# Linear attention and two expert layers on one core: the first four attention chunks with full-row instead of half-row matmuls from level 1 on

## Chip, cores and metric

One core of a Trainium2 chip (trn2). The metric is the time of one execution in microseconds of the device, from the first to the last instruction of the program with its start and end around it.

## What is computed

The program computes three layers on 4 x 768 tokens with model width 384, in fp32:

```python
# q, k, v, alpha: [4, 8, 768, 48]; state: [4, 8, 48, 48], zero at the start of each sequence
for t in range(S):
    state = alpha[:, :, t, :, None] * state + np.einsum('bhd,bhe->bhde', k[:, :, t], v[:, :, t])
    y[:, :, t] = np.einsum('bhd,bhde->bhe', q[:, :, t], state)
x = y, heads beside each other                    # [3072, 384]
h = x @ w_in; g = where(h > 0, h, exp(min(h, 0)) - 1); x = g @ w_out     # 384 -> 2048 -> 384
out = sum over e of p[:, e] * (maximum(x @ w1[e], 0) @ w2[e])            # 4 experts, 384 -> 1024 -> 384
```

## The kernel before, in words

**Units and chunks.** The 3072 tokens are 24 chunks of 128; two chunks are a unit. Channels lie on the partitions: a pair of heads takes 128 of them, each head 48 in a half of 64, the rest zero. Weights of the pairs (query t, key s inside a chunk) are found in seven levels: at level l, with h = 2^l, each block of 2h tokens gives the products of its right half's queries and its left half's keys, then the queries of the right halves and the keys of the left halves are multiplied by decays, so that the next level can use them. Decays of level l+1 are products of two of level l (`totals`, L1003, GpSimd).

**The first four chunks** (EARLY, units 0 and 1) come before anything else and have functions of their own; these are what the change touches. TensorE does `early_pairs` (L414), level by level, in each level chunks 0 to 3. For each of the four head pairs there are two matmuls, one per head, on the partitions 0 to 63 and 64 to 127 (a half of the rows each), 128 keys against the 64 right-half queries, into two PSUM banks (`ps_even`, `ps_odd`). Each fp32 matmul is two records in the trace, so a chunk is 16 records. VectorE does `early_queries` (L620, one multiply per unit and level, after both chunks of the unit) and, for levels 0 to 3, `early_masked` (L632): two predicated copies a chunk from PSUM into the weights. GpSimd does `early_keys` (L1029, one multiply per unit and level) and `totals`. ScalarE does levels 4 to 6 of the weights as `early_rectangles` (L827), 8, 4 and 2 small copies a chunk. A level of a chunk waits for queries, keys and the emptied bank of the level before.

**Behind the levels**, TensorE goes on in fixed order (L537 to L551): transposes of the keys (L449), the first state (L438), outer products (L461) and `attend` (L464, L479 and L481) for four chunks; ScalarE copies transposed keys (L856) and outputs into `x_tile` (L865, L867, L881). After attend 3 the expert layers start with the first 512 tokens: per weight block j (48 blocks a tile, six tiles) `hidden` and `output`, three fp32r matmuls (L500 to L502) of 512 columns per product. Weights are loaded by SP (L331), split into high and low parts by ScalarE (L874) and VectorE (L676). The other ten units of attention are spread over the blocks by the table PARTS_AT (L116); they already use full-row matmuls: queries are kept in slots (`QL`, [P, pair, 2, token]), the slot of head 0 with zeros below partition 63 and that of head 1 with zeros above, filled by `expand` (L806, L815), and one matmul of 128 columns serves a pair of heads (`pairs`, L399, L411).

**The queues.** SP issues every transfer in program order: alpha, keys, queries of unit 0 (512 KB each), masks, the same for unit 1, small constants, values, four weight blocks, the blocks of unit 2 (`load_blocks`), then `load_unit(2)`, whose waits for the key transposes and for attend 1 hold weights 4 to 7. The unit-1 queries lie in the buffer `p_rows`, the weights of chunk 2 in the other half of it, those of chunk 3 in `products`.

## Time and profile before

| | |
|---|---|
| median of 3 runs (lowest, highest) | 1410.71 us (1410.6, 1410.97) |
| the profiled execution's own time | 1410.88 us |
| its span, first to last instruction | 1409.1 us |
| TensorE matmul busy | 1386.8 us, 98% |
| TensorE weight load busy (beside it) | 1172.3 us, 83% |
| VectorE, ScalarE, GpSimd busy | 866.3 (61%), 664.7 (47%), 549.9 (39%) us |
| mean granted TensorE clock | 0.999 |
| 0 to 81 us: TensorE, VectorE, ScalarE, GpSimd busy | 70.15, 38.11, 26.66, 45.07 us |
| first matmul, first expert matmul | 7.48, 80.99 us |

The span is cut by the first and last instruction; the execution's time is 1.8 us longer. A row of the trace gives start or count, busy time and, in brackets, the idle time before it and who ended it. Matmul ends are modelled, so a busy TensorE is not one at its peak; for its speed look at how far apart the starts of like records lie, which in the chain of waits is the length given for a group.

### The profile page before, as it was taken

Reading aid. Unit: us, or ns where it says so; the run is one execution under the profiler, and the core shown is the slowest. Engines: PE = TensorE matmul, PEld = TensorE weight load, DVE = VectorE, ACT = ScalarE, POOL = GpSimd, SP = SyncE. Lnnn points to the kernel's source line nnn. Section 1 sums busy time; section 2 is a strip of 40 time slices with the busy share of each in tenths; the row PEclk is TensorE's granted clock in tenths of the full one; section 3 lists DMA queues with packets and bytes.
Section 4 is the critical chain, followed back from the end, with each engine's and each line's share of the span. In section 5 each row is a group of like instructions: output and inputs, shape, how many; then the busy total and the mean of one; then the engine's idle time right before and its main releaser. Section 6 shows DMA issues by size and latency. Waiting matters only on the chain.

```text
span 1409.1 us, 19709 instructions
## 1 busy us (share of the span) xinstructions
PE 1386.8 (98%) x6984; PEld 1172.3 (83%) x6984; DVE 866.3 (61%) x1199; ACT 664.7 (47%) x1187; POOL 549.9 (39%) x517
## 2 busy tenths in 40 slices
PE   7989999999999999999999999999999999999998
PEld 7978888888888888888888888888887888887886
DVE  5278777676556766556756646667655654654443
ACT  0556554436534446643444753443663443563331
POOL 6474383750443761155473153375134421100012
PEclk9999999999999999999999999999999999999999
DMA  5044434235435235424423523523542332343330
GB/s 224 16 160 152 124 103 157 68 88 181 146 91 187 84 90 166 158 79 145 136 79 96 196 91 112 180 80 95 172 152 85 91 97 79 118 126 92 99 101 23
DMA packets 84005, 166.21 MB, mean 118 GB/s; under 512 B 30146, under 2 KB 31683, under 8 KB 83908
## 3 DMA queue, kind: packets, MB, share of 16 engines
q1 hardware_dynamic: 83908, 164.96, 37.8%
q8 instruction: 56, 0.92, 0.3%
q14 instruction: 41, 0.34, 0.1%
HBM read 158.85 MB, written 6.08 MB: 117 GB/s over the span
## 4 chain that ended last, share of the span: by engine, by line
PE 89%; issue 5%; DVE 3%; ACT 2%; POOL 1%; DMA 1%; SPq 0%; POOLq 0%; ACTq 0%; DVEq 0%
PE ps_h L500 13%; PE ps_h L502 12%; PE ps_h L501 12%; PE ps_o L500 12%; PE ps_o L502 12%; PE ps_o L501 12%; PE ps_att L411 4%; PE ps_att L481 3%; PE ps_att L431 2%; PE ps_att L479 1%; PE ps_att L461 1%; PE ps_o L431 1%; DVE w_lo L676 1%; PE ps_att L449 1%; POOL acc L1056 1%
## 5 line engine op out<-in xcount | busy, mean ns | idle before, releaser
L500 PE MATMUL ps_o<-g_hi,w_lo 128*128 128x512 f32 x864 | 348.2, 403 | 1.2 <-DVE g_lo L692 1.2
L676 DVE TENSOR_TENSOR w_lo<-w_stage,w_hi 128x768 fp32r<-128x768 f32 x288 | 322.4, 1120 | 37.8 <-ACT w_hi L874 33.7
L500 PE MATMUL ps_h<-x_hi,w_lo 128*128 128x512 f32 x864 | 337.7, 391 | 7.3 <-DVE g_lo L696 3.7
L502 PE MATMUL ps_o<-g_hi,w_hi 128*128 128x512 f32 x864 | 337.5, 391 | 0.0
L501 PE MATMUL ps_o<-g_lo,w_hi 128*128 128x512 f32 x864 | 336.6, 390 | 0.0
L502 PE MATMUL ps_h<-x_hi,w_hi 128*128 128x512 f32 x864 | 336.4, 389 | 0.0
L501 PE MATMUL ps_h<-x_lo,w_hi 128*128 128x512 f32 x864 | 336.2, 389 | 0.0
L901 ACT ACTIVATE g_hi<-ps_h 128x512 fp32r<-128x512 f32 x192 | 114.8, 598 | 461.9 <-PE ps_h L502 461.2
L696 DVE SCALAR_TENSOR_TENSOR g_lo<-ps_h,g_hi 128x512 fp32r<-128x512 f32 x192 | 132.2, 689 | 235.7 <-ACT g_hi L901 235.4
L268 POOL TENSOR_TENSOR products<-q_block,k_block 128x384 f32<-128x384 f32 x150 | 190.9, 1286 | 136.9 <-DVE scores L613 134.2
L874 ACT CAST w_hi<-w_stage 128x768 fp32r<-128x768 f32 x288 | 239.0, 832 | 1.7
L500 PEld LDWEIGHTS ps_h<-x_hi,w_lo 128*128 128x128 f32 x864 | 162.1, 188 | 45.8 <-issue 6.2
L1056 POOL TENSOR_TENSOR acc<-acc,part 128x512 f32<-128x512 f32 x54 | 72.7, 1375 | 309.6 <-DVE part L722 309.6
L502 PEld LDWEIGHTS ps_o<-g_hi,w_hi 128*128 128x128 f32 x864 | 162.1, 188 | 35.7
L502 PEld LDWEIGHTS ps_h<-x_hi,w_hi 128*128 128x128 f32 x864 | 162.2, 188 | 34.1
L501 PEld LDWEIGHTS ps_h<-x_lo,w_hi 128*128 128x128 f32 x864 | 162.2, 188 | 33.4
L500 PEld LDWEIGHTS ps_o<-g_hi,w_lo 128*128 128x128 f32 x864 | 162.6, 188 | 31.6 <-DVE g_lo L692 2.0
L501 PEld LDWEIGHTS ps_o<-g_lo,w_hi 128*128 128x128 f32 x864 | 162.7, 188 | 30.0
L1027 POOL TENSOR_TENSOR k_level<-k_level,decay 128x256 f32<-128x256 f32 x60 | 39.1, 652 | 287.3 <-PE ps_att L411 287.3
L688 DVE SCALAR_TENSOR_TENSOR elu_out<-elu_exp,ps_h 128x512 f32<-128x512 f32 x96 | 65.8, 686 | 72.0 <-ACT elu_exp L890 72.0
L692 DVE TENSOR_TENSOR g_lo<-elu_out,g_hi 128x512 fp32r<-128x512 f32 x96 | 72.1, 752 | 61.1 <-ACT g_hi L896 61.1
L896 ACT CAST g_hi<-elu_out 128x512 fp32r<-128x512 f32 x96 | 59.6, 620 | 92.1 <-DVE elu_out L688 73.2
(101 smaller groups left out, 1404.4 us busy)
## 6 DMA issues: line engine op xcount, KB each, us to landing
w_stage<-in_w SPq DMA_DIRECT2D x288, 384.0 KB, 3.1
v_tok<-in_v SPq DMA_DIRECT2D x12, 576.0 KB, 5.0
alpha<-in_a SPq DMA_DIRECT2D x12, 512.0 KB, 4.1
k_level<-in_k SPq DMA_DIRECT2D x12, 512.0 KB, 6.1
p_rows<-p_norm SPq DMA_DIRECT2D x6, 1024.0 KB, 8.9
q_low<-in_q SPq DMA_DIRECT2D x11, 512.0 KB, 6.8
out<-acc SPq DMA_DIRECT2D x18, 256.0 KB, 4.3
q_block<-in_q_blocks SPq DMA_DIRECT2D x10, 384.0 KB, 3.7
```

The lines of the kernel that those rows point to most:

```text
L268: return engine.tensor_tensor(dst, q[:, :, 1, i:i + 1, :].broadcast_to([P, pairs, h, D]), k[:, :, 0], ALU.mult)
L500: nc.tensor.matmul(dst, lhs[1], rhs[0], start=first, stop=False)
L501: nc.tensor.matmul(dst, lhs[0], rhs[1], start=False, stop=False)
L502: return nc.tensor.matmul(dst, lhs[0], rhs[0], start=False, stop=last)
L676: nc.vector.tensor_tensor(wl[n % WRING][:], stage[n % STAGE][:], wh[n % WRING][:].bitcast(F32), ALU.subtract).then_inc(w_low, 1)
L688: nc.vector.scalar_tensor_tensor(gt[n % 2][:], ex[n % 2][:], -1.0, ps_h[n % 2][:], ALU.add, ALU.max).then_inc(h_read, 1)
L692: nc.vector.tensor_tensor(gl[n % GS][:], gt[n % 2][:], gh[n % GS][:].bitcast(F32), ALU.subtract).then_inc(g_ready, 1)
L696: nc.vector.scalar_tensor_tensor(gl[n % GS][:], ps_h[n % 2][:], 0.0, gh[n % GS][:].bitcast(F32), ALU.max, ALU.subtract).then_inc(g_ready, 1)
L874: nc.scalar.copy(wh[n % WRING][:], stage[n % STAGE][:]).then_inc(w_hi, 1)
L896: nc.scalar.copy(gh[n % GS][:], gt[n % 2][:]).then_inc(g_hi, 1)
L901: nc.scalar.activation(gh[n % GS][:], ps_h[n % 2][:], ACT.Relu).then_inc(g_hi, 1)
L1056: nc.gpsimd.tensor_tensor(acc[:, m, :], acc[:, m, :], part[k % 2][:], ALU.add).then_inc(acc_added, 1)
```

## The change

For the first four chunks, level 0 stays as it is. Levels 1 to 6 use the slot form: ScalarE copies the dense queries of a unit into zeroed slots after each query update (`early_slots`, the whole of both halves at level 0, only the changed right halves later), and TensorE does one full-row matmul of 128 columns for each pair, 8 records a chunk, into one bank. The predicated copies take 512 columns in one instruction from level 1 on, and level 4 is a masked copy on VectorE instead of small copies on ScalarE; levels 5 and 6 are 2 and 1 copies of ScalarE a chunk. VectorE clears `p_rows` as well, which becomes unit 1's slots; its dense queries move to `acc`, the first key and value to `part`, chunk 2's weights to the block buffers. Keys and queries are loaded by chunk (256 KB each, rows of 512 bytes) in the order chunk 0, alpha 0, chunk 1, masks, alpha 1, chunks 2 and 3. `load_unit(2)` stands ahead of `load_blocks(2)`, which waits for attend 2 (the third), since its buffer holds the weights of chunk 2; weights 4 to 7 are behind both. The diff, without renamed semaphores, index changes and the host's masks:

```diff
+MASKED = 5
...
-        blocks = [sb(f"{name}_block", [P, SUB * D]) for name in "qka"]
+        blocks = sb("blocks", [P, 3, SUB * D])
...
-        mk = sb("masks", [P, LOW, HALF])
-        k0 = acc[0:1, 0, :].rearrange("p (a t) -> p a t", a=PAIRS)
-        v0 = acc[0:1, 1, 0:PAIRS * 2 * D].rearrange("p (a e) -> p a e", a=PAIRS)
-        flat = pb[:].rearrange("p e t -> p (e t)")
-        QE = [QT[:], flat[:, 0:PAIRS * UNIT].rearrange("p (a t) -> p a t", a=PAIRS)]
-        PE_W = [PW[0][:], PW[1][:], flat[:, PAIRS * UNIT:2 * PAIRS * UNIT].rearrange("p (a t) -> p a t", a=HEADS),
-                prods[:].rearrange("p r x -> p (r x)")[:, 0:HEADS * P].rearrange("p (a t) -> p a t", a=HEADS)]
+        mk = sb("masks", [P, MASKED, HALF])
+        k0 = part[0][0:1, :].rearrange("p (a t) -> p a t", a=PAIRS)
+        v0 = part[1][0:1, 0:PAIRS * 2 * D].rearrange("p (a e) -> p a e", a=PAIRS)
+        QE = [QT[:], acc[:].rearrange("p a t -> p (a t)")[:, 0:PAIRS * UNIT].rearrange("p (a t) -> p a t", a=PAIRS)]
+        QS = [QL[:], pb[:].rearrange("p e (s t) -> p e s t", s=2)]
+        PE_W = [PW[0][:], PW[1][:]]
+        PE_W += [b[:].rearrange("p r x -> p (r x)")[:, 0:HEADS * P].rearrange("p (a t) -> p a t", a=HEADS) for b in (blocks, prods)]
...
+        q_in, e_in = sem("q_loaded"), [sem(f"early_q_k_loaded_{g}") for g in range(EARLY)]
@@ -261,7 +262,7 @@
@@ -282,31 +283,36 @@
             def load_blocks(u):
                 if u > LEAD:
                     sp.wait_ge(prod, NPROD * (u - LEAD))
+                else:
+                    sp.wait_ge(y_done, 3)
                 for i, d in enumerate((qb_d, kb_d, ab_d)):
-                    sp.dma_start(blocks[i][:], d[u]).then_inc(block_in[i], 16)
+                    sp.dma_start(blocks[:, i, :], d[u]).then_inc(block_in[i], 16)
 
             def load_unit(u):
                 s = u % 2
                 if u >= 2 * LEAD:
                     sp.wait_ge(k_low, LOW * (u - 2 - LEAD) + 1)
                     sp.wait_ge(q_low, LOW * (u - 2 - LEAD) + 1)
-                elif u >= LEAD:
+                else:
                     sp.wait_ge(e_k, early_unit(u - LEAD, 0))
                     sp.wait_ge(e_q, early_unit(u - LEAD, 0))
-                if u >= LEAD:
-                    sp.wait_ge(td_ready, LEVELS * (u - 2) + 1)
+                sp.wait_ge(td_ready, LEVELS * (u - 2) + 1)
                 sp.dma_start(TD[0][s][:], a_d[u]).then_inc(a_in[s], 16)
-                if u >= LEAD:
-                    sp.wait_ge(kt_done, 2 * (u - 1))
+                sp.wait_ge(kt_done, 2 * (u - 1))
                 sp.dma_start(KL[s][:], k_d[u]).then_inc(k_in[s], 16)
-                if u < LEAD:
-                    sp.dma_start(QE[u], q_d[u]).then_inc(e_q_in[u], 16)
-                    return
                 if u == LEAD:
                     sp.wait_ge(y_done, 2)
                 else:
                     sp.wait_ge(q_slots, u - LEAD)
                 sp.dma_start(QT[:], q_d[u]).then_inc(q_in, 16)
+
+            def load_early(g):
+                u, t = g // 2, slice(P * (g % 2), P * (g % 2 + 1))
+                sp.dma_start(KL[u][:, :, t], k_d[u][:, :, t]).then_inc(e_in[g], 16)
+                sp.dma_start(QE[u][:, :, t], q_d[u][:, :, t]).then_inc(e_in[g], 16)
+
+            def load_alpha(u):
+                sp.dma_start(TD[0][u][:], a_d[u]).then_inc(a_in[u], 16)
 
             def load_v(u):
                 if u >= 2:
...
 
-            load_unit(0)
+            load_early(0)
+            load_alpha(0)
+            load_early(1)
             sp.dma_start(mk[:], masks_d).then_inc(masks_in, 16)
-            load_unit(1)
+            load_alpha(1)
+            load_early(2)
+            load_early(3)
             sp.dma_start(k0, k0_d).then_inc(first_in, 16)
             sp.dma_start(v0, v0_d).then_inc(first_in, 16)
             sp.dma_start(eye[:], eye_d).then_inc(eye_in, 16)
@@ -354,8 +364,8 @@
             for n in range(STAGE):
                 load_w(n)
             sp.dma_start(pr_raw[:], probs_d).then_inc(p_raw_in, 16)
+            load_unit(LEAD)
             load_blocks(LEAD)
-            load_unit(LEAD)
             for n in range(STAGE, 2 * STAGE):
                 load_w(n)
             sp.wait_ge(p_step, 4)
@@ -413,27 +423,30 @@
 
             def early_pairs(g, l):
                 u, c = divmod(g, 2)
+                t = slice(P * c, P * (c + 1))
                 if l == 0:
-                    pe.wait_ge(k_in[u], 16)
-                    pe.wait_ge(e_q_in[u], 16)
-                else:
-                    pe.wait_ge(e_q, early_unit(u, l - 1))
+                    pe.wait_ge(e_in[g], 32)
+                else:
+                    pe.wait_ge(e_slot, early_unit(u, l - 1))
                     pe.wait_ge(e_k, early_unit(u, l - 1))
-                    if l <= LOW:
+                    if l <= MASKED:
                         pe.wait_ge(e_mask, early_chunk(g, l - 1))
                     else:
-                        pe.wait_ge(e_rect, early_chunk(g, l - 1 - LOW))
-                t = slice(P * c, P * (c + 1))
+                        pe.wait_ge(e_rect, early_chunk(g, l - 1 - MASKED))
                 for pr in range(PAIRS):
-                    for sd, ps_g in enumerate((ps_even[g], ps_odd[g])):
-                        r = slice(HALF * sd, HALF * (sd + 1))
-                        right = QE[u][r, pr, t].rearrange("p (m two h) -> p m two h", two=2, h=1 << l)[:, :, 1, :]
-                        last = nc.tensor.matmul(ps_g[:, HALF * pr:HALF * (pr + 1)], KL[u][r, pr, t], right, start=True, stop=True)
+                    if l == 0:
+                        for sd, ps_g in enumerate((ps_even[g], ps_odd[g])):
+                            r = slice(HALF * sd, HALF * (sd + 1))
+                            right = QE[u][r, pr, t].rearrange("p (m two) -> p m two", two=2)[:, :, 1]
+                            last = nc.tensor.matmul(ps_g[:, HALF * pr:HALF * (pr + 1)], KL[u][r, pr, t], right, start=True, stop=True)
+                    else:
+                        right = QS[u][:, pr, :, t].rearrange("p s (m two h) -> p s m two h", two=2, h=1 << l)[:, :, :, 1, :]
+                        last = nc.tensor.matmul(ps_even[g][:, pr * P:(pr + 1) * P], KL[u][:, pr, t], right, start=True, stop=True)
                 last.then_inc(e_step, 1)
 
             def first_state():
                 pe.wait_ge(first_in, 32)
-                pe.wait_ge(e_rect, early_chunk(0, LEVELS - 1 - LOW))
@@ -634,11 +647,16 @@
                 dve.wait_ge(e_step, early_chunk(g, l))
                 if l:
                     dve.wait_ge(e_mask, early_chunk(g, l - 1))
-                for sd, ps_g in enumerate((ps_even[g], ps_odd[g])):
-                    dst = weights(g).rearrange("p (a s) (m two h) -> p s a m two h", s=2, two=2, h=h)[:, sd, :, :, 1, :]
-                    mask = mk[:, l, :].rearrange("p (m h) -> p m h", h=h).unsqueeze(1).broadcast_to([P, PAIRS, HALF // h, h]).bitcast(U32)
-                    src = ps_g[:, 0:PAIRS * HALF].rearrange("p (a m h) -> p a m h", a=PAIRS, h=h)
-                    last = nc.vector.copy_predicated(dst, mask, src)
+                mask = mk[:, l, :].rearrange("p (m h) -> p m h", h=h).unsqueeze(1)
+                if l == 0:
+                    for sd, ps_g in enumerate((ps_even[g], ps_odd[g])):
+                        dst = weights(g).rearrange("p (a s) (m two) -> p s a m two", s=2, two=2)[:, sd, :, :, 1]
+                        last = nc.vector.copy_predicated(dst, mk[:, 0, :].unsqueeze(1).broadcast_to([P, PAIRS, HALF]).bitcast(U32),
+                                                         ps_g[:, 0:PAIRS * HALF].rearrange("p (a m) -> p a m", a=PAIRS))
+                else:
+                    dst = weights(g).rearrange("p a (m two h) -> p a m two h", two=2, h=h)[:, :, :, 1, :]
+                    last = nc.vector.copy_predicated(dst, mask.broadcast_to([P, HEADS, HALF // h, h]).bitcast(U32),
+                                                     ps_even[g][:].rearrange("p (a m h) -> p a m h", a=HEADS, h=h))
                 last.then_inc(e_mask, 1)
...
 
-            for buffer in (QL, SC[0], SC[1]):
+            for buffer in (QL, pb, SC[0], SC[1]):
                 nc.vector.memset(buffer[:], 0.0).then_inc(q_clear, 1)
...
                 for u in range(LEAD):
                     early_queries(u, l)
-                    if l < LOW:
+                    if l < MASKED:
                         for c in range(2):
                             early_masked(2 * u + c, l)
-            dve.wait_ge(q_clear, 3)
+            dve.wait_ge(q_clear, 4)
@@ -824,16 +842,29 @@
                     last = nc.scalar.copy(QD[g % 2][r, :, 0:HALF], QL[r, :, sd, P * (g % 2):P * (g % 2) + HALF])
                 last.then_inc(q_left, 1)
 
+            def early_slots(u, l):
+
+                act.wait_ge(e_q, early_unit(u, l))
+                if l:
+                    act.wait_ge(e_slot, early_unit(u, l - 1))
+                else:
+                    act.wait_ge(q_clear, u + 1)
+                for sd in range(2):
+                    r = slice(HALF * sd, HALF * (sd + 1))
+                    new, old = QS[u][r, :, sd, :], QE[u][r]
+                    if l:
+                        new, old = [x.rearrange("p a (m two h) -> p a m two h", two=2, h=1 << l)[:, :, :, 1, :] for x in (new, old)]
+                    last = nc.scalar.copy(new, old)
+                last.then_inc(e_slot, 1)
+
             def early_rectangles(g, l):
                 h = 1 << l
                 act.wait_ge(e_step, early_chunk(g, l))
                 act.wait_ge(cleared, CLEARS)
-                for sd, ps_g in enumerate((ps_even[g], ps_odd[g])):
-                    src = ps_g[:, 0:PAIRS * HALF].rearrange("p (a t) -> p a t", t=HALF)
-                    dst = weights(g).rearrange("p (a s) t -> p s a t", s=2)[:, sd]
-                    for m in range(HALF // h):
-                        last = nc.scalar.copy(dst[2 * m * h:(2 * m + 1) * h, :, (2 * m + 1) * h:(2 * m + 2) * h],
-                                              src[2 * m * h:(2 * m + 1) * h, :, m * h:(m + 1) * h])
+                src = ps_even[g][:].rearrange("p (a t) -> p a t", t=HALF)
+                for m in range(HALF // h):
+                    last = nc.scalar.copy(weights(g)[2 * m * h:(2 * m + 1) * h, :, (2 * m + 1) * h:(2 * m + 2) * h],
+                                          src[2 * m * h:(2 * m + 1) * h, :, m * h:(m + 1) * h])
                 last.then_inc(e_rect, 1)
...
-            for l in range(LOW, LEVELS):
-                for g in range(EARLY):
-                    early_rectangles(g, l)
+            for l in range(LEVELS):
+                for u in range(LEAD):
+                    if l >= MASKED:
+                        early_rectangles(2 * u, l)
+                    if l < LEVELS - 1:
+                        early_slots(u, l)
+                    if l >= MASKED:
+                        early_rectangles(2 * u + 1, l)
```

## Rows read from the trace of the kernel before

**Rows 1.** The page: granted clock of TensorE in 40 slices, tenths of full speed.

```profile
PEclk9999999999999999999999999999999999999999
```

**Rows 2.** The chain of waits from 0 to 110 us: start us, us, what.

```profile
13.75 1.75 PE ps_o L431 x17
...
56.46 1.04 PE ps_att L449 x4
57.50 1.95 PE ps_h L438 x8
...
60.49 3.57 PE ps_h L461 x16
...
65.77 0.43 PE ps_att L479 x2
...
71.28 1.76 PE ps_o L461 x16
...
80.99 0.47 PE ps_h L500
...
81.70 0.23 PE ps_h L502
```

**Rows 3.** The waits from 8 to 57 us: us in total, times, longest us.

```profile
DVE q_low L630 <- PE ps_h L431: 16.7, 7, 7.7
```

**Rows 4.** Weight loads, L461 and L431: ns min/median/max, first and last start us.

```profile
L461 PEld LDWEIGHTS ps_h<-v_tok,k_tok x16: 285/333/333, 60.3 to 63.5; 128*128 128x128 f32 x16
...
L461 PEld LDWEIGHTS ps_o<-v_tok,k_tok x16: 190/192/192, 71.0 to 72.7; 128*128 128x128 f32 x16
...
L431 PEld LDWEIGHTS ps_h<-q_low,k_level x112: 283/330/330, 7.5 to 52.5; 64*128 64x128 f32 x112
```

**Rows 5.** The chain of waits from 140 to 260 us: start us, us, what.

```profile
153.21 0.89 PE ps_att L411 x8
...
185.38 0.44 PE ps_att L449 x4
```

**Rows 6.** DMA issues (median us to landing), then order of time, query loads.

```profile
p_rows<-in_q SPq DMA_DIRECT2D x1, 512.0 KB, 8.1
...
3.57 0.45 SPq L303 DMA_DIRECT2D p_rows<-in_q  x1
...
11.82 0.44 PE L431 MATMUL ps_att<-p_rows,k_level 64*128 64x64 f32 x1 [0.66 <-DMA p_rows<-in_q]
```

**Rows 7.** VectorE in order of time, masks of levels 1 and 3: start us, us.

```profile
20.18 0.78 DVE L641 COPY_PREDICATED pair_weights<-masks,ps_h 128x256 f32<-128x256 uint32 x1
20.76 0.78 DVE L641 COPY_PREDICATED pair_weights<-masks,ps_att 128x256 f32<-128x256 uint32 x1
...
33.64 0.42 DVE L641 COPY_PREDICATED pair_weights<-masks,ps_h 128x256 f32<-128x256 uint32 x1
```

**Rows 8.** ScalarE: line L815, duration ns min/median/max, then the order of time.

```profile
L815 ACT COPY q_level<-q_low x20: 1035/1047/1052, 113.9 to 1102.2; 64x1024 f32<-64x1024 f32 x20
...
79.62 0.51 ACT L881 CAST x_hi<-x_tile 128x384 fp32r<-128x384 f32 x1
...
87.93 0.82 ACT L874 CAST w_hi<-w_stage 128x768 fp32r<-128x768 f32 x1
```

**Rows 9.** GpSimd in order of time; lines L981, L603 (ns min/median/max).

```profile
53.22 1.56 POOL L1039 TENSOR_TENSOR k_level<-k_level,decay 128x512 f32<-128x512 f32 x1 [1.85 <-PE ps_h L431]
...
99.74 1.60 POOL L268 TENSOR_TENSOR products<-q_block,k_block 128x384 f32<-128x384 f32 x1 [4.00 <-DVE scores L613]
...
L981 POOL TENSOR_TENSOR k_level<-k_level,decay x30: 1092/1556/2029, 81.7 to 1063.1; 128x512 f32<-128x512 f32 x30
...
L603 DVE TENSOR_TENSOR q_low<-q_low,alpha x10: 681/1418/1508, 94.1 to 1077.5; 128x512 f32<-128x512 f32 x10
```

**Rows 10.** SP in order of time, and a DMA issue (median us to landing).

```profile
71.68 5.85 SPq L331 DMA_DIRECT2D w_stage<-in_w  x4
...
a_block<-in_a_blocks SPq DMA_DIRECT2D x10, 384.0 KB, 5.7
```

More of the change, by code:

```diff
@@ L207, in program @@
         ps_even, ps_odd = [*ps_a, ps_o[1]], [*ps_h, ps_o[0], ps_o[2]]
-        q_in, e_q_in = sem("q_loaded"), [sem(f"early_q_loaded_{s}") for s in range(2)]
+        q_in, e_in = sem("q_loaded"), [sem(f"early_q_k_loaded_{g}") for g in range(EARLY)]
         block_in = [sem(f"block_{c}_loaded") for c in "qka"]
         masks_in, e_step, e_q, e_k = sem("masks_loaded"), sem("early_pairs_done"), sem("early_q_updated"), sem("early_k_updated")
-        e_mask, e_rect = sem("early_pairs_masked"), sem("early_pairs_rect")
+        e_slot, e_mask, e_rect = sem("early_q_in_slots"), sem("early_pairs_masked"), sem("early_pairs_rect")
         prod, change, red = sem("product"), sem("block_changed"), sem("reduced")
@@ L263, in block_op @@
             h, pairs = 1 << l, SUB >> l + 1
-            q, k, a = [x.rearrange("p (m two h) d -> p m two h d", two=2, h=h) for x in [b[:].rearrange("p (t d) -> p t d", d=D) for b in blocks]]
+            q, k, a = [x.rearrange("p (m two h) d -> p m two h d", two=2, h=h) for x in [blocks[:, b, :].rearrange("p (t d) -> p t d", d=D) for b in range(3)]]
             left, right = [a[:, :, side, 0:1, :].broadcast_to([P, pairs, h, D]) for side in range(2)]
@@ L435, in first_state @@
                 pe.wait_ge(first_in, 32)
-                pe.wait_ge(e_rect, early_chunk(0, LEVELS - 1 - LOW))
+                pe.wait_ge(e_rect, early_chunk(0, LEVELS - 1 - MASKED))
                 for pr in range(PAIRS):
@@ L443, in transpose_k @@
                     pe.wait_ge(e_k, early_unit(g // 2, LEVELS - 1))
-                    pe.wait_ge(e_rect, early_chunk(g, LEVELS - 1 - LOW))
+                    pe.wait_ge(e_rect, early_chunk(g, LEVELS - 1 - MASKED))
                 else:
@@ L976, in low_keys @@
                 else:
-                    pool.wait_ge(k_in[s], 16 * (u // 2 + 1))
+                    pool.wait_ge(k_in[s], 16 * (u // 2))
                     pool.wait_ge(a_in[s], 16 * (u // 2 + 1))
@@ L1118 @@
     step = np.arange(P)
-    masks = np.zeros((P, LOW, HALF), np.float32)
-    for l in range(LOW):
+    masks = np.zeros((P, MASKED, HALF), np.float32)
+    for l in range(MASKED):
         h = 1 << l
```

2 lines of the change are left out of this document (1 added, 1 removed).

## The prediction

> **What bounds the kernel now.** The page comes first. TensorE is busy 98% of the span and full to the edge from 90 us on, so a change to the first 80 us pays only by letting the expert layers start earlier. That makes the chain of waits in the first 81 us the second view. It is TensorE alone: matmuls of L431 from 7.5 to 56.46, transposes, first state and outer products to 65.77, the four attends, and the first expert matmul at 80.99 [rows 2]. The waits agree: VectorE stands seven times before the queries of unit 0, each time for TensorE [rows 3]. So the reader is to ask why TensorE needs 1.71 us for the 16 records of a chunk (17 records: 1.75 us).
>
> The third view is the length of one instruction in two stretches. A 128-column fp32 weight load takes 333 ns in the outer products at 60 to 64 us, 192 ns in the same line at 71 us; the half-row loads of L431 take 330 ns over their whole stretch [rows 4]. In the chain, 16 records of L461 take 3.57 us at 60.49 and 1.76 us at 71.28 [rows 2]. The page shows a granted clock of 9 (tenths of full speed, 90% or more) in every slice [rows 1]; the durations do not fit it. I go by the durations: TensorE runs at its lower level (1.2 GHz) until about 66 us and at the upper (2.4 GHz) after it, and 49 us of half-row matmuls without a gap did not lift it, while full-row ones did within some 5 us of 60.49. A full-row level chunk (L411) costs 0.89 us at the upper level [rows 5], so about 1.79 at the lower.
>
> The Trainium skill (TensorE: Matmul & The Clock Gate, Part 3) speaks against this change: small contractions packed in separate row groups run concurrently, the whole array being no faster per product. The rows agree at equal clock (1.71 against 1.79 for a chunk); by that rule alone the 24 changed chunks would cost 1.9 us more. The gain hangs on the clock.
>
> **The change, part by part.** The profiled execution took 1410.88 us, 0.17 above the median of the three runs; sums are against it.
>
> *Loads.* Before, the second query load, issued at 3.57, lands 8.1 us later, and chunk 2 starts at 11.82; chunks 2 and 3 end level 0 at 11.82 + 3.42 = 15.24 [rows 6]. After, the same bytes are queued up to the last key and query pair, though in 11 issues instead of 7 (0.45 us each, 5 us in all, inside the 11 us). Bandwidth sets the landing, so I keep 11.8, but only chunk 3 is left behind it: level 0 ends at 13.5. Rows of 512 bytes instead of whole partitions could be slower; bounds: landing at 9 (chunks then run through) and at 14.7.
>
> *Level 1.* Four full-row chunks at the lower clock, 7.1 us, if the slots are filled in time. The slot copies of level 0 are two of 64x1024, 1.05 us each [rows 8]; unit 1's end near 16.5, before TensorE reaches them at 17.1. TensorE is thus dense with full rows from 13.5; with the 5 to 6 us seen after 60.49 the clock rises near 19.5, and level 1 ends at 20.3.
>
> *VectorE.* A level-1 mask copy of 256 columns is followed by the next after 0.58 us; a level-3 one takes 0.42 instead of 0.78, and is followed after 0.33 [rows 7]. No row has 512 columns in one; 1.10 and 0.61 (double, less one fixed part) lie between 0.6 (if the short run length was the cost) and 1.16. Level 1 gives VectorE four masks and two query updates (0.61 each, the 0.68 of [rows 9] less a like overlap): 5.6 us from 17.4, to 23.0. The last mask holds back chunk 3 of level 2, which ends at 24.4.
>
> *Levels 3 to 6.* TensorE needs only 4 x 0.89 = 3.6 us a level; VectorE at most 2 x 0.61 + 4 x 0.61 = 3.7; GpSimd two key updates of 1.56 and a small decay, 3.4. What ends last is one unit's loop: two chunks 1.78, handover 0.25, queries 0.69, two slot copies of 64x512 (no row; between the 0.51 of 384 and the 0.82 of 768 elements [rows 8], 0.62 each, 1.15 for both, since the second starts before the first ends), handover 0.1: 4.0 us. There is a slower form of that loop. A VectorE query update that meets a running GpSimd operation takes up to 1.51 us instead of 0.68, and the key update is 1.56 in the early levels, where both start together, and 1.09 at its shortest later [rows 9]: the two take turns. If GpSimd goes first, its 1.09 stands ahead of the queries: some 5.0 us a level. VectorE, just finished with masks, will be late about as often as not: 4.6. Four levels: 24.4 + 18.4 = 42.8, bounds 40.4 and 44.4. Before, this point was 56.46: 13.7 us saved, bounds 12.1 and 16.1. The mask of level 4 moves from ScalarE to VectorE inside that sum.
>
> *Between levels and attend.* Before, 9.3 us of TensorE without a gap [rows 2]. After, all at the upper clock: transposes 4 x 0.44 [rows 5], first state 0.95 (half of its present 1.95), outer products 1.76, together 4.5. Work that was hidden by the slow clock appears: the level-6 rectangles of chunk 0 before the first transpose (0.8) and, behind the last rectangles, the key token copies (0.4). 5.7 us: 3.6 saved; bounds 2.4 (waits double) and 4.4 (almost none).
>
> *Attends and expert start.* Already at the upper clock: unchanged, 15.2 us from 65.77 to 80.99.
>
> *SP queue.* load_blocks now waits for the third attend, and behind it stand weights 4 to 7, issued from 71.68 on before [rows 10]. In the old time frame weight 4 would be issued near 77.1, after 1.15 MB of blocks. At 5.7 us to landing it is there at 83; ScalarE wants it at 87.93 [rows 8]. Cost nothing; were the 5 us of cover gone, each late us would count fully. The blocks land some 3 us after the fourth attend, which alone released GpSimd's first product before; GpSimd later waits 4.0 us for VectorE's scores [rows 9], which absorbs it. GpSimd's shifted operations meet VectorE elsewhere at 80 to 90: I give this plus or minus 1.5. The added memset of p_rows ends near 5.5, before anything needs VectorE.
>
> Sum: 13.7 + 3.6 = 17.3, so 1410.9 - 17.3 = **1393.6 us**.
>
> **The rivals.** *The clock stays low.* If half-zero operands in the slots, and not only half rows, keep the level down, 24 chunks cost 1.79: 13.5 + 42.9 = 56.4, the old 56.46, and the rest as before: 1411. For it: 49 us of dense work without a rise. Against: the same array rows, weights and columns as in L461, which rose. 7 in 100.
>
> *The clock rises and falls again.* The loop leaves TensorE idle up to 1.4 us in 5. If that brings the lower level back, a level costs 7.1 instead of 4.6: two such levels give 1398.6; all four and a low clock behind them (3.6) 1407. Against: the upper clock survives 2.7 us without a matmul before 80.99, where matmuls of 512 columns then start 0.23 us apart [rows 2]. 6 in 100, at 1403. The Trainium skill (same page, HAM oscillation) states that gaps between bursts bring the lower clock back; the trace's 2.7 us gap did not, so no run here shows it.
>
> *The loads are late, and the clock low* (slower). Place: chunk 3's pair of loads in small rows. Price: at half the rate of before, its 2 MB take 5 us more; level 1 starts at 18.5 and ends the levels at 61.4, with the low clock 5 us behind: 1416. It needs both; with a low clock it decides once the last pair lands after 14.6. 2 in 100. With the high clock the same lateness only shrinks the gain to about 12.
>
> *The two engines do not take turns* (no port between them): 4.0 a level, 40.4, so 1391.2. This is inside the forecast's range, as is 5.0 a level, 1395.2.
>
> **How the numbers follow.** The forecast has 85 in 100; the three others 7, 6 and 2 (the unsettled turns lie within the first). Its own bounds: best 16.1 + 4.4 = 20.5, 1390.4; worst 12.1 + 2.4, less 1.5 at the expert start, 13.0, 1397.9; a landing a little late adds one more, 1399. The range 1390.3 to 1399 leaves out the low clock and most of the falling clock, some 18 in 100. A measurement of this kernel can tell about 0.2%, 2.8 us, from no change. Faster by more: 0.85 plus 0.06, so 0.91; within: the low clock, 0.06 of its 0.07; slower 0.03, the last 0.01 with the late loads.
>
> **What would show it.** Right: in the chain of the new profile, L411-like chunks of 8 records at 1.79 us in level 1 and 0.89 from level 2 on; first expert matmul at 63 to 65 us; from there to the end the same as before within 1.5 us; levels 3 to 6 spaced 4 to 5 us, TensorE waiting for ScalarE's slots. Wrong: level chunks of 1.79 to the end (clock); TensorE waiting for masks beyond level 2 (VectorE) or for GpSimd's keys; ScalarE waiting for weight 4; the first chunks starting later than 7.5 (loads).

## The result, and the profile after

The changed kernel takes 1401.01 us (median of 4 runs, 1400.07 to 1401.96), the one before 1410.65 in the same comparison: 0.9928 of it, 95% interval 0.9913 to 0.9943, or 9.6 us less. It is faster, as forecast, but by little more than half of the 17.3, and the range (1390.3 to 1399) was missed by 2 us. The profiled execution took 1401.96 us, the longest of the four; its span is 1400.2.

The chain of waits of the changed kernel (start us, us, what; L441 are the half-row matmuls, L444 the full-row ones), to be held against [rows 2]:

```profile
6.01 8.12 DMA acc<-in_q
14.17 0.47 PE ps_att L441
...
17.85 3.72 PE ps_att L444 x16
...
50.52 0.44 PE ps_att L462 x4
...
55.36 0.44 PE ps_o L462 x4
...
70.62 0.47 PE ps_h L513
```

| point | before | forecast | after |
|---|---|---|---|
| level 1 begins | 15.24 | 13.5 | 17.85 |
| level 1 ends | | 20.3 | 23.5 |
| level 2 ends | | 24.4 | 29.4 |
| level 6 ends | 56.46 | 42.8 | 50.5 |
| first attend | 65.77 | 48.5 | 55.8 |
| first expert matmul | 80.99 | 63.7 | 70.62 |
| first L411 chunk (L421 after) | 153.21 | 135.9 | 144.26 |
| end of span | 1409.1 | 1391.8 | 1400.2 |

The ends of levels 1 and 2 are the start of their last chunk plus 0.9. Read by differences, the table tells where the 8.4 us between 1393.6 and the profiled 1402.0 lie: loads +4.35, level 1 -1.15, level 2 +1.8 (the two levels together +0.65), levels 3 to 6 +2.7, transposes to attend -0.4, attends -0.4, the expert start +1.4. Behind 144 us nothing changed: 1256 us to the end in both. The loads' share is that of one execution: the six profiled executions with loads by chunk (this one, e1, e4, e9, e10, e11) begin level 1 between 16.5 and 17.8 us, 17.1 in the mean, and this one is the latest.

**The loads.** SP of the changed kernel in order of time:

```profile
6.01 1.40 SPq L312 DMA_DIRECT2D acc<-in_q  x1
7.45 1.87 SPq L311 DMA_DIRECT2D k_level<-in_k  x1
...
9.36 0.83 SPq L312 DMA_DIRECT2D acc<-in_q  x1
```

Its DMA issues (KB each, median us from issue to landing), the queries of chunks 2 and 3:

```profile
acc<-in_q SPq DMA_DIRECT2D x2, 256.0 KB, 7.2
```

Its stretches 4 to 6 and 6 to 8 us (length, busy us of PE, PEld, DVE, ACT and POOL with instructions, granted clock, DMA share, GB/s):

```profile
4.00:6.00 2.00, 0.12 (x2) 0.12 (x2) 1.71 (x3) 0.36 (x1) 1.41 (x4) 1.00 1.01 176
6.00:8.00 2.00, 1.85 (x16) 1.66 (x16) 0.00 (x0) 0.00 (x0) 0.00 (x0) 1.00 0.95 296
```

The same stretches of the kernel before:

```profile
4.00:6.00 2.00, 0.00 (x0) 0.00 (x0) 0.00 (x0) 0.51 (x1) 1.96 (x5) 1.00 1.01 358
6.00:8.00 2.00, 0.52 (x6) 0.55 (x6) 0.00 (x0) 0.78 (x1) 1.76 (x4) 1.00 1.06 410
```

An issue takes up to 1.87 us where it took 0.45 [rows 6], and 176 and 296 GB/s move where 358 and 410 did. The transfer in the chain, issued at 6.01, is that of chunk 2's queries: it lands at 14.1 and chunk 2 starts then. Chunk 3's queries are issued at 9.36 and, if 7.2 is the mean of 8.1 and theirs, take 6.3 us and land near 15.6, before TensorE is done with chunk 2. So two chunks, not one, are left behind the wait, and the level ends at 17.85.

**The levels.** TensorE of the changed kernel in order of time in level 3 (start us, us, in brackets the idle before and who ended it):

```profile
30.15 2.05 PE L444 MATMUL ps_att<-q_level,k_level 128*128 128x128 f32 x16 [0.57 <-ACT q_level L857]
32.78 1.16 PE L444 MATMUL ps_att<-p_rows,k_level 128*128 128x128 f32 x8 [0.58 <-ACT p_rows L857]
...
35.34 2.05 PE L444 MATMUL ps_att<-q_level,k_level 128*128 128x128 f32 x16 [0.52 <-ACT q_level L857]
```

Beside it, in the same order and kernel, unit 0's keys on GpSimd, its queries on VectorE and its two slot copies on ScalarE, a fence for each engine:

```profile
32.37 1.09 POOL L1075 TENSOR_TENSOR k_level<-k_level,decay 128x512 f32<-128x512 f32 x1 [1.48 <-PE ps_att L444]
```

```profile
32.57 1.44 DVE L643 TENSOR_TENSOR q_low<-q_low,decay 128x512 f32<-128x512 f32 x1
```

```profile
34.05 1.25 ACT L857 COPY q_level<-q_low 64x512 f32<-64x512 f32 x2 [1.32 <-DVE q_low L643]
```

From unit 0's level 3 to its level 4 are 5.19 us. GpSimd starts the keys at 32.37, VectorE comes from its masks at 32.57 and its query update lasts to 34.0, the two slot copies to 35.3, and TensorE waits for them: the slower form of the loop. Unit 0's query update is slow in every one of levels 3 to 5 (1.40 to 1.44 us), not in half of them, and unit 1's in levels 1 to 4 (1.34 to 1.52).

**The expert start.** GpSimd of the changed kernel in order of time at the blocks of unit 2:

```profile
71.42 1.02 POOL L269 TENSOR_TENSOR products<-blocks 128x384 f32<-128x384 f32 x1 [3.59 <-DMA blocks<-in_a_blocks]
```

VectorE in the same view, two subtractions of the low weights and a query update of unit 2:

```profile
79.31 1.92 DVE L694 TENSOR_TENSOR w_lo<-w_stage,w_hi 128x768 fp32r<-128x768 f32 x1
...
84.55 1.85 DVE L694 TENSOR_TENSOR w_lo<-w_stage,w_hi 128x768 fp32r<-128x768 f32 x1
...
88.69 1.51 DVE L616 TENSOR_TENSOR q_low<-q_low,decay 128x512 f32<-128x512 f32 x1
```

TensorE in the same view, its two long waits between 81 and 146 us:

```profile
109.84 0.50 PE L513 MATMUL ps_h<-x_hi,w_lo 128*128 128x512 f32 x1 [0.93 <-DVE elu_out L706]
...
137.44 0.50 PE L513 MATMUL ps_o<-g_hi,w_lo 128*128 128x512 f32 x1 [0.78 <-DVE g_lo L710]
```

### The profile page after: what moved, and what is told of

It is laid out like the page before. It is cut to its first block, busy times and chain, and to the rows that moved or that the text cites. A ratio compares the mean times of both kernels' runs of the same rounds, so it can differ in the third digit from the quotient of the medians.

```text
span 1400.2 us, 19310 instructions
## 1 busy us (share of the span) xinstructions
PE 1368.5 (98%) x6792; PEld 1151.7 (82%) x6792; DVE 874.6 (62%) x1192; ACT 673.0 (48%) x1167; POOL 548.7 (39%) x517
## 4 chain that ended last, share of the span: by engine, by line
PE 86%; issue 5%; DVE 4%; ACT 2%; POOL 1%; DMA 1%; SPq 0%; POOLq 0%; DVEq 0%; ACTq 0%
PE ps_h L513 13%; PE ps_h L515 13%; PE ps_h L514 13%; PE ps_o L513 12%; PE ps_o L515 12%; PE ps_o L514 12%; PE ps_att L421 4%; PE ps_att L494 3%; PE ps_att L492 1%; PE ps_att L474 1%; DVE w_lo L694 1%; PE ps_att L462 1%; POOL acc L1092 1%; DVE elu_out L706 1%; DMA acc<-in_q 1%
## 5 line engine op out<-in xcount | busy, mean ns | idle before, releaser
L269 POOL TENSOR_TENSOR products<-blocks 128x384 f32<-128x384 f32 x150 | 191.3, 1289 | 136.7 <-DVE scores L626 130.8
L1092 POOL TENSOR_TENSOR acc<-acc,part 128x512 f32<-128x512 f32 x54 | 72.8, 1377 | 309.5 <-DVE part L740 309.5
```

What stands on the lines that cost most here:

```text
L269: return engine.tensor_tensor(dst, q[:, :, 1, i:i + 1, :].broadcast_to([P, pairs, h, D]), k[:, :, 0], ALU.mult)
L1092: nc.gpsimd.tensor_tensor(acc[:, m, :], acc[:, m, :], part[k % 2][:], ALU.add).then_inc(acc_added, 1)
```

## The experiments

Each was run beside the kernel before (medians 1410.45 to 1410.63). Gains are told from the 1401.0 of the changed kernel, which gave 1401.29 when it was run again (e9).

**Keys behind the queries** (e1):

```diff
 pool.wait_ge(e_step, early_chunk(2 * u + 1, l))
+pool.wait_ge(e_q, early_unit(u, l))
```

> Levels 3 to 6 of the changed kernel take 5.2 us each, and in each the GpSimd key update (1.05 to 1.15 us) runs ahead of the VectorE query update, which then takes 1.4 to 1.5 us instead of 0.69. Theory (turns): the two engines take turns, and the key update, which nobody waits for, goes first because VectorE is late with masks. With the key update made to wait for the query update of the same unit and level, the query update falls to about 0.7 everywhere, the slots come 0.8 us sooner, and a level takes 4.0 to 4.4 us: level 6 ends 3 to 4.5 us sooner, the time is 1397 to 1398. Rival (VectorE is full): masks and queries fill VectorE, and the query update is long because of its own strides; then a level stays at 5.2 and the time at 1401.

1397.51 us (0.9907, 0.9892 to 0.9922). The query updates of the changed kernel by line (count, shortest/median/longest ns, from and to in us):

```profile
L643 DVE TENSOR_TENSOR q_low<-q_low,decay x6: 692/1062/1439, 21.7 to 47.9; 128x512 f32<-128x512 f32 x6
L643 DVE TENSOR_TENSOR acc<-acc,decay x6: 691/1422/1520, 24.6 to 50.7; 128x512 f32<-128x512 f32 x6
```

The same lines of this kernel:

```profile
L643 DVE TENSOR_TENSOR q_low<-q_low,decay x6: 692/693/742, 20.5 to 43.2; 128x512 f32<-128x512 f32 x6
L643 DVE TENSOR_TENSOR acc<-acc,decay x6: 691/714/767, 23.3 to 46.0; 128x512 f32<-128x512 f32 x6
```

Its TensorE in order of time, in levels 3 to 5:

```profile
28.36 2.02 PE L444 MATMUL ps_att<-q_level,k_level 128*128 128x128 f32 x16 [0.66 <-POOL k_level L1076]
...
32.59 2.02 PE L444 MATMUL ps_att<-q_level,k_level 128*128 128x128 f32 x16 [0.28 <-ACT q_level L857]
...
36.79 2.03 PE L444 MATMUL ps_att<-q_level,k_level 128*128 128x128 f32 x16 [0.26 <-ACT q_level L857]
```

Median 1062 and 1422 ns become 693 and 714, and a level 4.2 us. VectorE does the same work on the same views; so it was the turns, not a full VectorE. They cost 3.5 us of the run. This execution also began level 1 sooner (16.66 against 17.78, in TensorE's order of time), which the edit does not explain; from there to the transposes it took 29.0 us against 32.6, so the levels alone gained 3.6.

**Loads by unit** (e2): keys and queries of a unit in one transfer each, keys, queries, alpha; PE waits for both at its first chunk.

```diff
-sp.dma_start(KL[u][:, :, t], k_d[u][:, :, t]).then_inc(e_in[g], 16)
-sp.dma_start(QE[u][:, :, t], q_d[u][:, :, t]).then_inc(e_in[g], 16)
+sp.dma_start(KL[u][:], k_d[u]).then_inc(e_in[2 * u], 16)
+sp.dma_start(QE[u], q_d[u]).then_inc(e_in[2 * u], 16)
...
 load_early(0)
 load_alpha(0)
+sp.dma_start(mk[:], masks_d).then_inc(masks_in, 16)
 load_early(1)
-sp.dma_start(mk[:], masks_d).then_inc(masks_in, 16)
 load_alpha(1)
-load_early(2)
-load_early(3)
```

> In the changed kernel level 0 ends at 17.6 us, before it ended at 15.2. Theory (small rows): keys and queries by chunk are 512-byte rows, SP's issues stretch to 0.6 to 1.9 us and the transfers move 176 to 296 GB/s between 4 and 8 us, where the kernel before moved 358 to 410. With keys and queries loaded by unit, 4 transfers instead of 8, whole partitions, the order otherwise kept, level 0 ends near 15.2 or sooner, though chunk 0 starts later (near 7), and the time is 1398.5 to 1399.5. Rival (order or bytes alone): the last pair is late because all 3 MB stand ahead of it, whatever the rows; then level 0 ends at 17 or later and the time stays at 1401.

1399.19 us (0.9921, 0.9904 to 0.9937). Level 1 begins at 14.75 in the chain of waits, before the 15.24 of the kernel before, and the first matmul is at 5.71 against 5.88. Over the profiled executions, level 1 begins at 13.7 to 14.7 (14.1 in the mean of e2, e5, e6, e8) with loads by unit and at 17.1 in the mean with loads by chunk: 2.9 us. That is not the price of the small rows alone. Alpha 1 (512 KB) stood ahead of the loads of chunks 2 and 3 and stands behind unit 1's here, and there are 4 issues instead of 8. At the 391 to 405 GB/s that the kernel before moved from 8 to 12 us, 512 KB are some 1.3 us (an estimate), so about 1.6 are left for rows and issues, which no run separates. So the expectation's "the order otherwise kept" does not hold, and its rival (order or bytes) is refuted only in part. Loading by chunk started chunk 0 only 0.4 us sooner (5.3 against 5.7 in the mean of the same executions).

In the profiled pair the first expert matmul comes 3.1 us sooner (67.54 against 70.62) and the end of the span 2.6; the medians differ by 1.8, because the profiled execution of the changed kernel was the longest of its four. In this execution the clock had fallen in the gap before the first expert matmul (TensorE in order of time):

```profile
67.54 0.77 PE L510 MATMUL ps_h<-x_hi,w_lo 128*128 128x512 f32 x1 [2.59 <-DVE x_lo L697]
68.11 0.63 PE L511 MATMUL ps_h<-x_lo,w_hi 128*128 128x512 f32 x1
68.53 0.63 PE L512 MATMUL ps_h<-x_hi,w_hi 128*128 128x512 f32 x1
```

Stretches of the same execution, the granted clock third from the end:

```profile
68.00:70.00 2.00, 2.00 (x6) 1.52 (x6) 0.43 (x2) 0.00 (x0) 1.26 (x2) 0.50 0.98 379
...
71.00:72.00 1.00, 1.00 (x6) 0.80 (x5) 0.00 (x0) 0.75 (x2) 1.00 (x2) 1.00 0.80 252
```

**Half rows at the upper clock** (e3, e12): the kernel before with full-row matmuls on a zeroed buffer ahead of chunk 0 (14, both) and ahead of chunk 2 (16, the second only). The edit of the second:

```diff
+pe.wait_ge(cleared, 4)
+for i in range(14):
+    nc.tensor.matmul(ps_even[0][:, 0:P], PE_W[3][:, 0, :], PE_W[3][:, 1, :], start=True, stop=True)
 for l in range(LEVELS):
     for g in range(EARLY):
+        if l == 0 and g == 2:
+            for i in range(16):
+                nc.tensor.matmul(ps_even[2][:, 0:P], PE_W[3][:, 0, :], PE_W[3][:, 1, :], start=True, stop=True)
         early_pairs(g, l)
```

> The kernel before with 14 full-row fp32 matmuls of 128 columns on a zeroed buffer ahead of its first chunk, while TensorE would wait for the loads (2.7 to about 8 us). Theory (half rows do not lift the clock but may hold it): the dummies raise it, and the half-row chunks then cost 0.85 instead of 1.71 us; if that holds for all 28 chunks, VectorE and the loops bound the levels and the time falls by 12 to 20 us, below the changed kernel. Theory (half rows do not count as work): the clock falls back some microseconds after the last dummy, chunks return to 1.71, and the time is within 3 us of 1410.7. Rival (zero operands do not raise it): chunks are 1.71 from the first, and the time is 1411 to 1412.

> The kernel before, warmed as in the earlier run, and with 16 more full-row matmuls in front of chunk 2, so that TensorE comes to the half-row chunks of levels 0 to 6 at the upper level and without a pause (in the earlier run it had been idle from 9.3 to 11.5 us before the clock fell at 12.8). At the upper level a half-row chunk cost 0.89 us there (pairs 0.11 us apart), as much as a full-row one. Theory (half rows neither lift nor hold the clock): it falls again within some microseconds of the last full-row matmul, chunks go from 0.89 to 1.71, and the time is 1409 to 1411. Rival (only the pause made it fall; dense half rows hold it): the clock stays, the levels are bound by VectorE and the loops, and the time is below 1400.

1409.14 us (0.9992, 0.9982 to 1.0001) and 1411.24 (1.0009, 0.9999 to 1.0019). TensorE of the first (e3) in order of time:

```profile
7.71 0.27 PE L431 MATMUL ps_att<-q_low,k_level 64*128 64x64 f32 x1
7.72 0.27 PE L431 MATMUL ps_h<-q_low,k_level 64*128 64x64 f32 x1
7.82 0.27 PE L431 MATMUL ps_att<-q_low,k_level 64*128 64x64 f32 x1
```

Stretches of the first (e3), the granted clock third from the end:

```profile
12.00:13.00 1.00, 1.00 (x19) 1.00 (x18) 0.67 (x2) 0.00 (x0) 0.63 (x1) 0.80 1.02 419
...
20.00:40.00 20.00, 20.00 (x192) 20.00 (x191) 12.79 (x28) 3.26 (x16) 10.86 (x10) 0.50 0.11 44
...
64.00:70.00 6.00, 6.00 (x58) 6.00 (x56) 1.96 (x4) 4.56 (x10) 0.83 (x1) 1.00 0.00 0
```

Stretches of the second (e12):

```profile
17.00:18.00 1.00, 1.00 (x23) 1.00 (x22) 1.00 (x2) 0.00 (x0) 1.00 (x1) 1.00 1.04 369
18.00:20.00 2.00, 1.51 (x28) 1.40 (x26) 2.00 (x5) 0.00 (x0) 2.00 (x2) 1.00 1.03 395
20.00:21.00 1.00, 1.00 (x19) 0.92 (x18) 1.00 (x3) 0.00 (x0) 1.00 (x2) 1.00 1.05 412
21.00:22.00 1.00, 0.44 (x6) 0.25 (x3) 1.00 (x3) 0.00 (x0) 0.68 (x2) 0.50 0.82 324
...
20.00:40.00 20.00, 19.26 (x188) 19.02 (x186) 14.46 (x32) 2.03 (x10) 10.06 (x10) 0.53 0.11 41
```

With the clock raised, the pairs of half-row records are 0.11 us apart, 0.89 a chunk, just as full rows; with the clock low, 0.21. So the zero operands raised the clock. The first kernel waits 2.1 us for chunk 2 (9.4 to 11.6) and loses the clock at 12.6 (0.80 is the mean of 0.6 us at 1.00 and 0.4 at 0.50). The second comes dense with full rows to 14.8, goes on dense with half rows to 18.6, pauses 0.49 us there, and loses it at 21.0. The full rows of the changed kernel keep it with two such pauses (0.5 to 0.6 us) in each level from 3 to 5, and through one of 1.27 us in level 2. From the fall to near 64 us TensorE of the first kernel is full, and that of the second but for one wait of 0.74 us at 21.4, and both stay at 0.50. So 40 us of dense half rows did not lift the clock, and half rows with one pause of 0.49 us did not hold it; the form of the change does both. Whether half rows without any pause would hold it was not tried. Nor was it separated what in the form matters: a half-row matmul also has 64 columns where a full-row one has 128, and writes its pair into two banks.

In these two traces the clock column shows the low stretch, which the page of the kernel before shows as 9. In every trace here the column has 1.00 up to its first change, also while the matmuls are at the slow pace (level 1 of the changed kernel, the half rows of the kernel before); the likely reading, which no run tests, is that the column starts at 1.00 and follows only recorded changes.

**Blocks of unit 2 early** (e4), chunk 2's weights in the buffer of the exponent:

```diff
+exs = sb("elu_exp", [P, 2, TILE])
...
-PE_W += [b[:].rearrange("p r x -> p (r x)")[:, 0:HEADS * P].rearrange("p (a t) -> p a t", a=HEADS) for b in (blocks, prods)]
+PE_W += [b.rearrange("p r x -> p (r x)")[:, 0:HEADS * P].rearrange("p (a t) -> p a t", a=HEADS) for b in (exs[:], prods[:])]
...
-else:
-    sp.wait_ge(y_done, 3)
...
+load_blocks(LEAD)
 load_unit(LEAD)
-load_blocks(LEAD)
```

> The changed kernel gained 10.4 us up to the first expert matmul and lost 1.4 of it by 144 us: two waits of TensorE, 0.93 and 0.78, that the kernel before had not. Theory (blocks late): GpSimd waits 3.6 us for the blocks of unit 2, its updates then meet VectorE's low-weight subtraction (1.85 to 1.92 us instead of 0.9) where it is needed. With chunk 2's weights in the exponent buffer, the blocks loaded at the start as before and ahead of unit 2, both waits go and the time falls by 1 to 1.5 us, to 1399.7. Rival (position only): the waits come from how VectorE, ScalarE and GpSimd stand to each other 10 us earlier, whatever the blocks do; then the time stays within 0.5 us of 1401.

1399.78 us (0.9924, 0.9909 to 0.9938). The waits at 110 and 137 us are gone. Because the clock differed between the profiled executions, the comparison was repeated with the gap filled (below).

**Together** (e5), and **with the gap filled** (e6: 8 full-row matmuls on the identity before `hidden_ready(0)`):

```diff
+pe.wait_ge(xa_ready, 1)
+for i in range(8):
+    nc.tensor.matmul(ps_even[0][:, 0:P], eye[:], eye[:], start=True, stop=True)
 for n in range(AHEAD):
     hidden_ready(n)
```

> The three edits together: key updates wait for the query updates (alone 1397.5), keys and queries loaded by unit (alone 1399.2), blocks of unit 2 loaded at the start (alone 1399.8); the changed kernel is 1401.0. If they act on three separate stretches, as I hold, the gains add: 1401.0 - 3.5 - 1.8 - 1.2 = 1394.5, level 1 starting near 14.5 and levels 4.2 us apart. If two of them share a cause, the time is 1396 or more. The low clock found in two of the runs at the first expert matmuls (0.77 us for the first instead of 0.47, granted clock 0.50 for 3.4 us) may add up to 1.5.

> The same with 8 full-row matmuls on the identity in the 2.6 us in which TensorE waits for the first tile between the last attend and the first expert matmul. Theory (the gap can drop the clock): the granted clock stays 1.00 through the expert start in every run, the first expert matmuls are 0.23 us apart from the start, and the time is 0.5 to 1.5 us below the one without them, with less spread. Rival (the fall is harmless, since VectorE and ScalarE bound the expert start): same time within 0.3 us, though the clock stays up.

1393.83 us (0.9878, 0.9863 to 0.9893) and 1393.28 (0.9876, 0.9861 to 0.9890). The three gains add: 3.5 + 1.8 + 1.2 = 6.5 expected, 7.2 from 1401.0. The filler brings 0.5, at the edge of what can be told: the two sets of runs overlap (1393.48 to 1393.93, 1393.00 to 1394.08).

**Fillers at the start too** (e7: e6 with 14 before chunk 0 and 8 before chunk 2):

> The same with fillers at the beginning too: 14 full-row matmuls before chunk 0 and 8 in the wait for chunk 2's loads. Theory (the clock of level 1 is the rest of the loss): if level 1 then starts at the upper level, its chunks cost 0.89 instead of 1.86 us, level 2 is reached up to 2.6 us sooner, and the time falls by 1 to 2 us. Rival (VectorE bounds levels 0 and 1 in any case: 5.6 us each for masks and queries): the chunks are short but level 2 comes less than 1 us sooner. Second rival: the half-row chunks of level 0 let the clock fall before level 1, as in the warmed kernel of before at 12.6 us, and nothing changes.

1392.82 us (0.9871, 0.9857 to 0.9886), the lowest median of all, 0.5 below e6, with runs that overlap its own. TensorE in level 1 and 2:

```profile
14.53 2.08 PE L440 MATMUL ps_att<-q_level,k_level 128*128 128x128 f32 x16
17.59 1.17 PE L440 MATMUL ps_att<-p_rows,k_level 128*128 128x128 f32 x8 [0.98 <-ACT p_rows L863]
...
19.93 2.08 PE L440 MATMUL ps_att<-q_level,k_level 128*128 128x128 f32 x16 [0.26 <-POOL k_level L1082]
```

Level 1's first two chunks take 2.0 instead of 3.7 us, so level 0's half rows did not lose the clock here. Yet level 2 begins at 19.93 against 19.78 in e6: TensorE then waits for slots and keys, as the rival has it. The test is not clean, for the fillers were also late: chunk 0 starts at 8.68 behind them where it started at 5.70 in e6, chunk 2 at 12.59 instead of 10.04, and level 1 at 14.53 instead of 13.65. Fillers that end in time might have shown up to 0.9 us more (an estimate from these starts).

**Level 4 back to ScalarE** (e8: e6 with MASKED = 4):

> The kernel with mends and filled gap, but level 4 of the weights is done by ScalarE's small copies again (4 a chunk, 0.2 us each) as in the kernel before, not as a masked copy of VectorE. Theory (VectorE is the tighter engine, so the move was not free but right): VectorE is freed of 2.4 us in level 4, ScalarE gets 16 copies, some 2.7 us for the four chunks, between its slot copies, which TensorE waits for: level 4 to 5 takes 5 to 6 us instead of 4.2 and the time is 1 to 1.5 us longer. Rival (VectorE bound): the level gets shorter and the time falls by 0.3 us or more.

1396.07 us (0.9895, 0.9879 to 0.9912), 2.8 longer than e6; the direction was right, but 1 to 1.5 was forecast. TensorE in levels 4 and 5 (here a unit's levels are 6.6 us apart):

```profile
34.47 2.31 PE L440 MATMUL ps_att<-q_level,k_level 128*128 128x128 f32 x16 [0.29 <-ACT q_level L856]
37.91 1.16 PE L440 MATMUL ps_att<-p_rows,k_level 128*128 128x128 f32 x8 [1.14 <-ACT p_rows L856]
...
41.03 2.05 PE L440 MATMUL ps_att<-q_level,k_level 128*128 128x128 f32 x16 [0.81 <-ACT q_level L856]
```

**What the expert start lost** (e9: the changed kernel; e10: with the gap filled; e11: with the gap filled and the blocks early; the edits are those of e4 and e6):

> The changed kernel itself, on the same chip as the next two, because the effects told apart here are about 1 us. 1400.5 to 1401.5, and the same two waits of TensorE near 110 and 137 us where the clock stays up.

> The changed kernel with 8 full-row matmuls on the identity in TensorE's last wait before the first expert matmul, nothing else. Theory (only some executions lose the clock there, and VectorE bounds the expert start): 0 to 0.6 us below the changed kernel, and a narrower spread. Rival (the clock's fall is the 1.4 us that the expert start lost): 1 us or more below.

> The changed kernel with the blocks of unit 2 loaded at the start and the gap filled. Theory (the late blocks are the 1.4 us): 1 to 1.5 us below the one with the filled gap alone, TensorE without the waits of 0.93 and 0.78 us at the exponent and at 137 us. Rival (the gain of the early blocks was another clock state or chip): equal to it within 0.4 us.

1401.29 us (0.9935, 0.9921 to 0.9948), 1401.01 (0.9932, 0.9920 to 0.9944) and 1399.78 (0.9923, 0.9909 to 0.9936). The blocks early bring 1.2 us, with runs that do not overlap (1400.37 to 1401.68, 1399.36 to 1400.23); the gap filled brings 0.3, which cannot be told from nothing. TensorE's waits of e10 between 90 and 170 us (us in total, times, longest):

```profile
PE ps_h L513 <- DVE elu_out L709: 0.9, 1, 0.9
PE ps_o L513 <- DVE g_lo L713: 0.8, 1, 0.8
```

The same view of e11:

```profile
PE ps_o L512 <- DVE g_lo L712: 0.3, 1, 0.3
```

In e9 the clock fell, and of the two waits expected there only one of 0.7 us is left. The time from the first expert matmul to the first full-row chunk between the blocks (L411 before) sorts all profiled executions:

| blocks of unit 2 | clock at the expert start | us |
|---|---|---|
| early | stays up (before, e3, e12, e6, e7, e8, e11) | 72.2 |
| early | falls (e4, e5) | 72.8 |
| late | stays up (after, e1, e10) | 73.6, 74.1, 74.0 |
| late | falls (e2, e9) | 74.1, 74.2 |

Late blocks cost 1.4 to 1.9 us there, whatever the clock does. The fall costs 0.6 where the blocks are early, as e6 gains on e5, and nothing that shows where they are late.

## Why the prediction was right in kind and wrong in size

**The clock** was read rightly from the durations, against the column: it carries the change. The low-clock price of a full-row chunk was 1.86 (3.72 for 16 records), forecast 1.79, and the rise came 4 us after the dense full rows began, not 6. Hence level 1 was 1.15 us shorter than forecast. "The clock stays low" did not happen. The Trainium skill (TensorE: Matmul & The Clock Gate, Part 3) has it that matmuls in separate row groups run concurrently. At equal clock this fits both levels: a chunk of half rows costs 0.89 against 0.89 and 1.71 against 1.86. It does not decide the outcome, because the clocks were not equal.

**The loads** are the first failed step: "Bandwidth sets the landing, so I keep 11.8, but only chunk 3 is left behind it: level 0 ends at 13.5." Chunk 2's queries alone landed at 14.1, chunk 3's near 15.6, two chunks were left behind the wait, and the level ended at 17.85 (16.5 to 17.8 in the six profiled executions). I took the bytes at the old rate for the price and the issues as hidden; from 4 to 8 us the queue moved 236 GB/s in the mean where it had moved 384, and issues stretched. The bound of 14.7 for the landing stood in the text, but it did not enter the worst case of 1397.9, and the 1 us that was added to reach 1399 is less than the 2.9 it would have cost. Loading by unit, with alpha 1 behind, takes 2.9 us off the start of level 1 and 1.8 off the time.

**Levels 3 to 6** are the second: VectorE "will be late about as often as not: 4.6". For unit 0 it was late every time in levels 3 to 5, 5.2 us a level, a little over the 5.0 that I had as a bound. (That its own delay sets the loop, and so brings the engines to the same phase again, is how I read it; it was not tried by itself.) Four levels cost 2.7 us more than forecast; e1 gives 3.5 back, since it also helps level 2.

**Levels 1 and 2**: 1.10 for a mask of 512 columns was right (1.15 from start to start); forgotten was that the query update behind the late masks meets GpSimd too (1.34 us instead of 0.61). That is 0.7 us, the whole excess of the two levels together. The other 1.15 of level 2's 1.8 is only what level 1 had gained: VectorE, not TensorE, sets the end of level 2, as the forecast had it, so a shorter level 1 brings nothing.

**Slots**: 1.15 forecast, 1.25 measured. **Between levels and attend**: 5.7 forecast, 5.3. **Attends**: 15.2, 14.8. The last two took 0.8 us off a miss that would otherwise have been larger. In the working itself two figures do not come out of their terms, without effect on the forecast: level 1 would end at 20.1, not 20.3, and the cases that the range leaves out have at most 15 in 100 (7, 6 and 2), not 18.

**The SP queue** is the third: weight 4 was indeed hidden, but that GpSimd's later wait of 4.0 us "absorbs" the late blocks was wrong. GpSimd's first product waited 3.6 us for the blocks, and what follows it met VectorE elsewhere. Counted from the first expert matmul, VectorE is 0.2 us behind the kernel before when it is done with the low-weight subtraction at 84.55, and 1.4 behind one block later (its next steps start at 86.33 and 91.44, in the kernel before at 96.47 and 100.37), where a remainder `g_lo` takes 1.07 instead of 0.69 and the query update at 88.69 takes 1.51 instead of 0.69; VectorE is what TensorE waits for in these blocks. I had given plus or minus 1.5 and zero for the value; e11 prices it at 1.2, and the trace at 1.4 to 1.9.

**The falling clock** as a rival was judged by one row: 2.7 us idle without a fall [rows 2]. Nine profiled executions have that gap unfilled (2.6 to 2.7 us). In e2 and e4 the clock fell in it, in e5 and e9 some 1.5 and 1.3 us behind it, each time to 0.50 for 3.4 us; in the kernels before and after, e1, e3 and e12 it did not fall. The Trainium skill (TensorE: Matmul & The Clock Gate, HAM oscillation) has it that gaps between bursts of matmuls bring the lower clock back: four executions agree, five do not. What decides it is not shown. It costs at most 0.6 us here, not the 5 of the rival, because VectorE bounds the expert start. My sentence that no run shows it no longer holds.

## What to carry to other kernels

Ask of a full TensorE at which clock it is full: the same form in two stretches tells (333 and 192 ns here), and matmuls in the half-row form can be dense for 40 us without lifting the clock to the upper level. Once TensorE is made faster, write down for each loop of the other engines who starts first: an operation nobody waits for, started 0.2 us ahead on an engine that takes turns with the critical one, cost 0.8 us each time, and one wait removed it. A load split to start sooner has to be priced by its row length, its issues and what stands ahead of it, not by its bytes alone. One profiled execution is one sample: the same loads began level 1 anywhere within 1.3 us, so compare stretch with stretch, not end with end.

## What the runs showed of the hardware

Half-row fp32 pairs run 0.11 us apart at the upper and 0.21 at the lower clock (e3), as fast per chunk as full rows at the same level. Dense half-row pairs did not lift the clock in 40 us (e3, e12). Full-row matmuls on zeros raise the clock (e3). With keys and queries in 512-byte rows and twice the issues, 176 to 241 GB/s moved from 4 to 6 us and 265 to 337 from 6 to 8 in the six profiled executions, where whole partitions moved 358 and 410 in the kernel before; an issue on SP took up to 1.87 us instead of 0.45. Row length and number of issues were not separated. A VectorE update of 128x512 that meets a GpSimd operation already running takes 1.3 to 1.5 us, with the order turned round 0.69 (e1). A predicated copy of 512 columns with runs of two elements takes 1.15 us from start to start, with runs of four or more 0.61. After the same gap of 2.6 to 2.7 us the clock fell in four executions of nine. The clock column of a trace shows 1.00 ahead of its first change, also where the durations are those of the lower clock.
